# First query loads moved behind the last key loads, weight chunks of GpSimd tied to attention units, query transposes in two row halves

## What is computed

```python
# q, k, v: batch 4, heads 8, seq 576, head_dim 64;  w_phi: 64 x 128
def phi(x):
    proj = np.einsum('bhsd,df->bhsf', x, w_phi)
    proj = proj - np.max(np.abs(proj), axis=-1, keepdims=True)
    return np.concatenate([np.exp(proj), np.exp(-proj)], axis=-1)
q_p, k_p = phi(q), phi(k)
kv  = np.einsum('bhsf,bhsd->bhfd', k_p, v)
z   = np.sum(k_p, axis=2)
num = np.einsum('bhsf,bhfd->bhsd', q_p, kv)
den = np.einsum('bhsf,bhf->bhs', q_p, z)[..., None] + 1e-06
x = num / den                    # 2304 tokens x 512
# dense layer: (silu(x @ w_gate) * (x @ w_val)) @ w_out, 512 -> 1536 -> 512
# then a choice of one of 8 experts for each token, relu(x @ w1[e]) @ w2[e], scaled
```

## Time and profile before

| | |
|---|---|
| median of 3 runs | 951.65 us (950.98 to 951.83) |
| the profiled execution | 954.05 us, its span 952.3 us |
| attention | start to 161.4 us |
| dense layer, then experts | 161.4 us to the end |
| PE busy | 896.0 us, 94% of the span |
| DVE, ACT, POOL busy | 371.9, 265.4, 157.5 us |
| chain that ended last | PE 87%, DMA 4%, SP's queue 2%, DVE 2%, issue 2% |

### The profile page before, as it was taken

The page is one execution under the profiler, slowest core; times in us unless marked ns, Lnnn a source line. Parts: engine busy times, 40 slices in busy tenths (PEclk is TensorE's granted clock), DMA queues, the critical chain, the costliest instruction groups (busy, mean ns, idle before and its releaser), DMA issues.

```text
span 952.3 us, 21360 instructions
## 1 busy us (share of the span) xinstructions
PE 896.0 (94%) x8032; PEld 803.9 (84%) x8033; DVE 371.9 (39%) x814; ACT 265.4 (28%) x484; POOL 157.5 (17%) x208
## 2 busy tenths in 40 slices
PE   8899999999999999999999999998559999999994
PEld 5788898989999898998989899897448888888883
DVE  4567786322224142221314223236544222624521
ACT  4465444212222121222212121125123112523321
POOL 6775000700000000000000000000113222332221
PEclk9899999999999999999999999999679999999997
DMA  9986442400010000001000000005411112415110
GB/s 242 272 216 201 133 124 80 123 12 34 1 45 0 34 10 11 33 0 44 0 23 22 11 33 0 23 1 199 181 41 44 44 44 77 177 37 203 50 34 18
DMA packets 64207, 68.44 MB, mean 72 GB/s; under 512 B 32415, under 2 KB 48927, under 8 KB 64161
## 3 DMA queue, kind: packets, MB, share of 16 engines
q1 hardware_dynamic: 57600, 45.21, 15.6%
q0 software_dynamic: 6560, 22.56, 7.7%
HBM read 54.11 MB, written 14.69 MB: 72 GB/s over the span
## 4 chain that ended last, share of the span: by engine, by line
PE 87%; DMA 4%; SPq 2%; DVE 2%; issue 2%; ACT 0%; POOL 0%; POOLq 0%; DVEq 0%
PE bank L1058 33%; PE bank L1079 16%; PE bank L1201 10%; PE bank L1182 9%; PE bank L952 4%; PE bank L1027 4%; PE bank L976 3%; PE bank L1010 2%; PE bank L1194 2%; PE bank L1095 2%; DMA scale_rows<-r_scale 1%; PE bank L1088 1%; PE bank L1165 1%; DMA out<-o_sb,row_out 1%; DMA e_w<-w 1%
## 5 line engine op out<-in xcount | busy, mean ns | idle before, releaser
L739 DVE TENSOR_TENSOR prod<-silu,bank 128x256 f32<-128x256 f32 x108 | 45.5, 421 | 249.8 <-ACT silu L531 249.8
L1058 PE MATMUL bank<-x_hi,wg_hi 128*128 128x256 f32 x432 | 125.3, 290 | 0.0
L1058 PE MATMUL bank<-x_hi,wv_hi 128*128 128x256 f32 x432 | 122.3, 283 | 0.0
L1058 PE MATMUL bank<-x_lo,wv_hi 128*128 128x256 f32 x432 | 122.3, 283 | 0.0
L1058 PE MATMUL bank<-x_hi,wv_lo 128*128 128x256 f32 x432 | 122.2, 283 | 0.0
L1058 PE MATMUL bank<-x_hi,wg_lo 128*128 128x256 f32 x432 | 122.2, 283 | 0.0
L1058 PE MATMUL bank<-x_lo,wg_hi 128*128 128x256 f32 x432 | 122.1, 283 | 0.0
L531 ACT ACTIVATE silu<-bank 128x256 f32<-128x256 f32 x108 | 41.6, 385 | 253.1 <-PE bank L1058 253.1
L1079 PE MATMUL bank<-wo_hi,h_hi 128*128 128x512 f32 x216 | 85.8, 397 | 0.0
L1079 PE MATMUL bank<-wo_hi,h_lo 128*128 128x512 f32 x216 | 84.3, 390 | 0.0
L1079 PE MATMUL bank<-wo_lo,h_hi 128*128 128x512 f32 x216 | 84.2, 390 | 0.0
(11 more groups left out here) (188 smaller groups left out, 1614.6 us busy)
## 6 DMA issues: line engine op xcount, KB each, us to landing
e_w<-w SPq DMA_DIRECT2D x32, 512.0 KB, 5.1
stage<-w_out POOLq DMA_DIRECT2D x16, 384.0 KB, 3.8
x_in<-x_rows SPq DMA_DIRECT2D x9, 512.0 KB, 3.6
y_rows<-y_sb SPq DMA_DIRECT2D x18, 256.0 KB, 2.0
k_sb<-kT SPq DMA_DIRECT2D x16, 256.0 KB, 5.7
v_sb<-v SPq DMA_DIRECT2D x16, 256.0 KB, 5.8
q_sb<-qT SPq DMA_DIRECT2D x16, 256.0 KB, 4.5
x_rows<-x_sb SPq DMA_DIRECT2D x16, 256.0 KB, 3.1
```

The lines of the kernel that those rows point to most:

```text
L739: dve.tensor_tensor(prod[:, c % 2, :], silu[:, c % 2, :], bank[2 + c % 2][:, 0:GT], ALU.mult).then_inc(prod_ready, 1)
L1058: mm = pe.matmul(acc[:, 0:GT], w[:, k, cols], x[:, k, :], start=(k == 0 and i == 0), stop=(k == KC - 1 and i == 2))
```

## The change

The five loads of batch 0's queries and the two of the router move in SP's list from behind the first batch's keys and values to behind those of the last batch. `load(n)` on POOL gets a second wait: chunk n (2 to 23) goes only once `4 * n // 3` units are projected. And `turn` does each transpose as two, of 64 tokens each, from the row halves of `dif` (partitions 0 to 63 and 64 to 127) to banks 2 and 3; features then lie as all first halves, all second halves, and `attend` reads them there.

```diff
             load_v(0, JF)
-            for j in range(JS):
-                load_q(0, j)
-            sp.dma_start(w_lg[:, :, 0:E], w_router).then_inc(wlg_in, 16)
-            sp.dma_start(w_lg[:, :, E:2 * E], w_outgate).then_inc(wlg_in, 16)
             ahead = KUNITS - JS
             for u in range(ahead + 2):
                 if u < ahead:
...
                     load_v((u - 2) // JS + 1, (u - 2) % JS)
+            for j in range(JS):
+                load_q(0, j)
+            sp.dma_start(w_lg[:, :, 0:E], w_router).then_inc(wlg_in, 16)
+            sp.dma_start(w_lg[:, :, E:2 * E], w_outgate).then_inc(wlg_in, 16)
...
             def load(n):
+                if not jobs[n][3] and n >= 2:
+                    pool.wait_ge(proj_done, 4 * n // 3)
                 pool.dma_start(stage[:, n % 2, :], jobs[n][0]).then_inc(w_raw[n % 2], 16)
...
-            def features(U, src):
-                n = heads(U % JS) * F
+            def features(U, src, dst):
...
-                    ins = act.activation(feat[:, U % 2, sign, 0:n], src[:, 0:n], ACT.Exp, scale=1.0 - 2 * sign)
+                    ins = act.activation(dst(feat[:, U % 2, sign]), dst(src), ACT.Exp, scale=1.0 - 2 * sign)
...
+            def by_token(U):
+                return lambda x: x[:, 0:heads(U % JS) * F]
+
+            def by_half(U):
+                return lambda x: x.rearrange("f (c t) -> f c t", c=2)[:, :, 0:heads(U % JS) * TAIL]
...
-                features(U, bank2[1])
+                features(U, bank2[1][:], by_half(U))
...
                 for h in range(n):
-                    mm = pe.transpose(bank2[1][:, h * P:(h + 1) * P], dif[:, U % 2, h * F:(h + 1) * F], ident[:])
+                    for half in range(2):
+                        rows = slice(half * TAIL, (half + 1) * TAIL)
+                        mm = pe.transpose(bank[2 + half][:, h * TAIL:(h + 1) * TAIL], dif[rows, U % 2, h * F:(h + 1) * F], ident[rows, rows])
...
-                                           feat[:, s, sign, i * P + half * TAIL:i * P + (half + 1) * TAIL],
+                                           feat[:, s, sign, half * 512 + i * TAIL:half * 512 + (i + 1) * TAIL],
```

More of the change, by code:

```diff
@@ L503, in features @@
                 for sign in range(2):
-                    ins = act.activation(feat[:, U % 2, sign, 0:n], src[:, 0:n], ACT.Exp, scale=1.0 - 2 * sign)
+                    ins = act.activation(dst(feat[:, U % 2, sign]), dst(src), ACT.Exp, scale=1.0 - 2 * sign)
                 ins.then_inc(exp_done, 1)
+            def by_token(U):
+                return lambda x: x[:, 0:heads(U % JS) * F]
+            def by_half(U):
+                return lambda x: x.rearrange("f (c t) -> f c t", c=2)[:, :, 0:heads(U % JS) * TAIL]
             for U in range(KUNITS):
                 act.wait_ge(dif_ready, U + 1)
-                features(U, dif[:, U % 2])
+                features(U, dif[:, U % 2], by_token(U))
                 if U % JS == 0 and U:
```

## The result

The change takes 943.61 us (median of 5 runs, 940.54 to 948.46) where the kernel before takes 951.65 (median of 5 as well, 950.98 to 951.83): a ratio of 0.992, 95% interval 0.990 to 0.994. That is faster by 0.8%, about half of the 1.64% forecast. The profiled execution is the slowest of the five, 948.46 us with a span of 946.7; it is 5.6 us under the profiled execution of before (954.05).

A forecast was written before the change was run, and what follows sets the result against it. PE, busy 94% of the span, was taken to bound the kernel, with DVE close behind in the query half. Terms 4.7 + 2.5 + 6.9 + 1.0 + 0.5 = 15.6 us off 951.65 gave 936.0, range 931.5 to 944.

The forecast's parts named there:

- The stall on batch 1's keys: Key half, PE's wait before batch 1's first project: moving the query loads saves 4.7 us, or 3.8 if keys land later.
- The clock: Key half, groups behind the long wait: without idle time PE keeps its full clock, saving 2.5 us.
- The transposes: Query turns: a pair of halves takes 58 ns against 107.5 for a whole transpose, saving 6.9 us in all.
- Rival 1: Turns: halves gain nothing because the load of 128 columns sets the pace; 943.9 us, chance 0.14.
- Between the phases: Border of project and turn: part of 0.23 us vanishes with equal tiles, saving 1.0 us, ends 0 and 2.7.
- both PE terms: Query half: the savings in transposes, 6.9 us, and at the border of project and turn, 1.0 us.
- The query loads moved: Query loads behind the last values: the first block lands with 1 to 2 us to spare, so cost 0.
- POOL's pace: POOL's new wait for projected units before weight chunks: own effect 0, with cover of tens of us.
- The issue gaps: Key half, PE's gaps put down to issue: a shorter queue removes some, saving 0.5 us, ends -1.5 and +2.3.
- if the issue gaps grow with the 144 added transposes: Named as a way the prediction would be wrong, beside the price of a pair; no size given.

The follow-up runs named there:

- e1: The kernel before with only the seven query and router loads moved, turns and weight chunks as before; 946.9 us, ratio 0.995 to the kernel before.
- e3: The change with its two router loads issued only after the attention; 941.51 us, ratio 0.989 to the kernel before.
- e5: The change again, unaltered, on the chip of e6 to e8; 942.81 us, ratio 0.991 to the kernel before.
- e4: The change without POOL's new wait for projected units; 941.55 us, ratio 0.9895 to the kernel before.
- e11: As e6, but weight chunk n waits for unit 3n up to n = 6 and 14 + n from there; 937.57 us, ratio 0.984.
- e12: e11's weight chunks with the change's own order of SP's loads, queries and router at once; 939.65 us, ratio 0.9865 to the kernel before.
- e6: The change with batch 0's query loads spread, one behind each of the last five key units, and router loads after the attention; 940.14 us, ratio 0.9895.
- e7: As e6, with every weight chunk from 2 on waiting for all 20 key units; 936.53 us, ratio 0.983 to the kernel before.
- e8: As e6, with weight chunk n behind unit min(2n, 32), half the change's density; 938.62 us, ratio 0.986 to the kernel before.
- e10: e7 with whole transposes: the kernel before with e6's edits on SP and e7's on POOL; 940.12 us, ratio 0.987 to the kernel before.
- e9: The kernel before with all weight chunks but the first two waiting for the last key unit; 944.51 us, ratio 0.991.

## Why the prediction was wrong in size

**The stall on batch 1's keys** (forecast 4.7): right. The wait is absent, and e1's key half is shorter by 7.2 us, which is 4.7 and the clock's 2.5.

**The clock** (2.5): right at its place, 1.16 and 2.09 us at full clock behind 21 us. But the prediction let it be lost only "if PE still stands idle as long as now", at that place. In the change's profiled run PE stood idle for 2.13 and 3.15 us elsewhere, and the half clock cost (1.67 - 1.16) + (3.13 - 2.09) = 1.55 us behind 45.16 and (2.08 - 1.16) + (3.73 - 2.09) = 2.56 behind 74.11: 4.1 us, more than was freed. The length of a stretch alone does not decide: behind 2.05 us (e3) and 2.01 (e5) groups were slow too, behind 2.33 (e4) none was, and of two stretches of 1.77 us that of e11 was followed by a slow group and that of e12 was not.

**The transposes** (6.9): right. A turn of 16 halves takes 0.59 us; it shrank by 0.43, forecast 0.40. A half's weight load lasts as long in the records as a whole one's did, 139 ns beside the 140 of the earlier trace rows:

```profile
L1019 PEld LDWEIGHTS bank<-ident,dif 64*128 64x128 f32 x288 | 11.3, 139 | 3.0 <-issue 2.6
```

But sixteen of them fit into 0.59 us, 37 ns each, so they do not run one after the other. The Trainium skill ("TensorE: Matmul & The Clock Gate", LDWEIGHTS) counts columns divided by 1.2 GHz, 107 ns. An estimate by that page is at least 0.86 us for eight pairs, even if the two loads of a pair run at once, and the trace does not agree for transposes. Rival 1 is out.

**Between the phases** (1.0) and DVE: of the 0.23 us at the border between `project` and `turn` 0.09 vanished, in 20 units 1.8 us; the upper end, the whole border, did not come. DVE takes some back: once a batch the unit behind the short attend takes 3.87 us instead of 3.61. The query halves without their gaps come to 71.0 to 72.0 us with halves (73.4 in e11, whose clock fell there) and 77.9 to 78.2 without, so both PE terms together gave 6 to 7 us for the 7.9 forecast. That is a mis-sized sum, off by 1 to 2 us.

**The query loads moved** (0) and **POOL's pace** (0): the pace is right (e4). For the loads the prediction had no cost at all. All queries landed in time, as it said. But behind their burst, 3.75 + 0.70 + 2.81 us of issues with nothing between, PE has a gap of 2.0 to 3.15 us in the change, e3, e4 and e5 and of 0.96 in e1; there is none in the five kernels that spread the loads (e6, e7, e8, e10, e11), and none in e12, which has the burst with fewer chunks beside it. No pair of medians prices it: e3 and e6 have the same ratio within their intervals, and so have e11 and e12. The early wait of 1.2 us for batch 0's third key block is in none of the terms either; e5, e7, e8, e10 and e12 have it too, 1.0 to 1.3 us, e3 and e4 do not, and its cause is open.

**The issue gaps** (0.5 gained, ends -1.5 and +2.3): this is the step that failed, in sign and beyond its lower end. It supposed that a shorter queue would thin the gaps. They grew in the profiled run from 4.7 to 8.2 us, and drew the clock with them, a cost that the term did not have at all. The profiled key halves close so: 4.69 and 2.46 freed; 2.48 of gaps, 1.0 of the early wait and 4.11 of clock lost; that is 0.4 us more lost than freed, while both key halves end at 82.53, so 0.4 us is not accounted for. In medians the change gained 8.0, where stall, clock and the query half give 4.7 + 2.5 + 6.5 = 13.7: 5.7 are missing. That gaps, early wait and clock took them is an estimate from the profiles; e7, without gaps in its key half, is 6.3 us below e5.

Two things make the packets late. The first is dense traffic: e7, e9 and e10 have no gap at 188 to 189 GB/s in the key half, with either order of queries and either form of transposes; kernels at 232 to 265 have 1.0 to 6.6 us, and the two between (213 and 219) have 1.7 and 0.6. The three quiet ones are also those without GpSimd's chunks in the key half, so no run separates the rate from the chunks' own queue. The second is a PE that comes sooner to the end of a block, since it works more instructions a us: a query unit was 2 x (16 + 8 + 64) = 176 of them in 4.13 us, 43 a us, and is 2 x (16 + 16 + 64) = 192 in 3.61 us, 53 a us. Halves save PE's time and add instructions. At like traffic in the query half whole turns have gaps of 0 (e10) and 0.92 us (e9), halves of 2.63 (e7), 3.40 (e11) and 2.97 (e12); that is one profile each, so the second point is less firm than the first. The prediction named this ("if the issue gaps grow with the 144 added transposes") and gave it no rival and no chance. Open stays what makes a single packet late: e11 has the longest query-half sum at a modest 207 GB/s, and e6 few at 263.

## What to carry to other kernels

A gap of PE that "issue" ends in a stretch with full transfer queues is a cost to plan for: compare the rate of transfers there and the number of instructions PE needs a microsecond, before crediting an edit that makes PE faster by more, smaller instructions. Loads that nobody awaits for tens of microseconds (here the dense layer's weights) belong where PE's instruction rate is lowest or other traffic is light. Whether a burst of loads should be spread the medians here leave open: five of the six profiles with the burst have a gap of 0.96 us or more behind it, none of the five that spread it. A stall removed gives the clock back only if no new idle stretch takes its place, so the clock's share has to be counted over the whole stretch, not at the old stall.

## What was not expected of the hardware

PE's program comes in packets of 16 KB, one for 256 instructions, through the same DMA engines as the data: at 53 instructions a us, one every 4.9 us. PE goes past the end of a block no sooner than 1.25 us after the packet has landed. With 264 GB/s in the key half of before, waits for packets took 4.0 us, with 189 GB/s for none (e7, e9, e10). The Trainium skill ("Runtime: NRT & Kernel Launch", Instruction fetch mechanics) has engines fetch their program in such blocks and calls the cost of a block's border mostly hidden. The size of a packet and the place of the gaps agree with it. Hidden the cost is not here: the change's attention has 8.2 us of such gaps.

Sixteen transposes of 64 rows ran in 0.59 us, 37 ns each, with 64 output columns on alternate row halves. And the key half's gaps took the clock to its 1.2 GHz level behind idle stretches of 2.13 and 3.15 us, as the stall of 4.69 us did; behind 0.48 us at 18.58 the groups kept their 2.09, and in e4 so they did behind 2.33.
